# First two units of the linear attention: level blocks of 64 keys, one unit two levels ahead of the other, decays on VectorE, x from PSUM

## The reference

```
for t in range(S):
    state = alpha[:, :, t, :, None] * state + np.einsum('bhd,bhe->bhde', k[:, :, t], v[:, :, t])
    y[:, :, t] = np.einsum('bhd,bhde->bhe', q[:, :, t], state)
...
h = x @ w_in                                   # 384 -> 2048
g = np.where(h > 0.0, h, alpha * (np.exp(np.minimum(h, 0.0)) - 1.0))
x = g @ w_out                                  # 2048 -> 384
...
p = domain_probs / (domain_probs.sum(-1, keepdims=True) + 1e-09)
for e in range(E):                             # 4 experts, 384 -> 1024 -> 384
    out += p[:, e:e + 1] * (np.maximum(x @ w1[e], 0.0) @ w2[e])
```

## Time and profile before

| | |
|---|---|
| Time, median of 3 | 1351.81 us |
| Profiled execution, its time | 1348.95 us |
| Its span | 1347.2 us |
| TensorE busy | 1296.9 us (96%) |
| VectorE / ScalarE / GpSimd busy | 832.6 / 605.9 / 564.3 us |
| TensorE in the 40 slices of the span | 2589999999999999999999999999999999999998 |

### The profile page before, as it was taken

The page is one execution under the profiler, slowest core; times in us unless marked ns, Lnnn a source line. Parts: engine busy times, 40 slices in busy tenths (PEclk is TensorE's granted clock), DMA queues, the critical chain, the costliest instruction groups (busy, mean ns, idle before and its releaser), DMA issues.

```text
span 1347.2 us, 27542 instructions
## 1 busy us (share of the span) xinstructions
PE 1296.9 (96%) x11112; PEld 1067.4 (79%) x11112; DVE 832.6 (62%) x1097; ACT 605.9 (45%) x1043; POOL 564.3 (42%) x485
## 2 busy tenths in 40 slices
PE   2589999999999999999999999999999999999998
PEld 2568788888888888888888888888888888888886
DVE  2478676675576766567676567666647654654443
ACT  0456534347534336733435753434754433653331
POOL 5574384840353861174691164484035321100012
PEclk9999999999999999999999999999999999999999
DMA  6054435236435335524424533523643333433330
GB/s 229 20 165 156 132 107 163 75 102 188 140 106 196 87 98 164 170 85 141 151 83 125 178 117 110 168 90 100 189 141 106 99 87 94 148 94 102 98 95 23
DMA packets 87682, 165.84 MB, mean 123 GB/s; under 512 B 30338, under 2 KB 35843, under 8 KB 87556
## 3 DMA queue, kind: packets, MB, share of 16 engines
q1 hardware_dynamic: 87556, 164.08, 39.4%
HBM read 157.97 MB, written 6.08 MB: 122 GB/s over the span
## 4 chain that ended last, share of the span: by engine, by line
PE 90%; issue 6%; DVE 1%; POOL 1%; DMA 0%; ACT 0%; SPq 0%; POOLq 0%; DVEq 0%; ACTq 0%
PE ps_o L563 14%; PE ps_h L563 14%; PE ps_o L564 14%; PE ps_o L565 14%; PE ps_h L564 14%; PE ps_h L565 14%; PE ps_att L438 2%; PE ps_att L532 1%; POOL acc L1075 1%; PE ps_att L508 1%; PE ps_att L536 1%; PE ps_att L490 1%; PE ps_att L541 1%; DMA alpha<-in_a 0%; PE ps_o L470 0%
## 5 line engine op out<-in xcount | busy, mean ns | idle before, releaser
L726 DVE TENSOR_TENSOR w_lo<-w_stage,w_hi 128x768 fp32r<-128x768 f32 x288 | 340.2, 1181 | 30.8 <-ACT w_hi L894 27.1
L563 PE MATMUL ps_o<-g_hi,w_lo 128*128 128x512 f32 x864 | 342.5, 396 | 0.7 <-DVE g_lo L742 0.7
L563 PE MATMUL ps_h<-x_hi,w_lo 128*128 128x512 f32 x864 | 338.2, 391 | 4.4 <-DVE x_lo L732 3.8
L921 ACT ACTIVATE g_hi<-ps_h 128x512 fp32r<-128x512 f32 x192 | 114.8, 598 | 500.0 <-PE ps_h L565 499.9
L564 PE MATMUL ps_h<-x_lo,w_hi 128*128 128x512 f32 x864 | 337.0, 390 | 0.0
L565 PE MATMUL ps_h<-x_hi,w_hi 128*128 128x512 f32 x864 | 337.0, 390 | 0.0
L564 PE MATMUL ps_o<-g_lo,w_hi 128*128 128x512 f32 x864 | 336.7, 390 | 0.0
L565 PE MATMUL ps_o<-g_hi,w_hi 128*128 128x512 f32 x864 | 336.6, 390 | 0.0
L746 DVE SCALAR_TENSOR_TENSOR g_lo<-ps_h,g_hi 128x512 fp32r<-128x512 f32 x192 | 132.3, 689 | 262.8 <-ACT g_hi L921 262.6
L894 ACT CAST w_hi<-w_stage 128x768 fp32r<-128x768 f32 x288 | 239.4, 832 | 1.0
L272 POOL TENSOR_TENSOR products<-blocks 128x384 f32<-128x384 f32 x150 | 194.8, 1312 | 90.6 <-DVE scores L673 88.2
(11 more groups left out here) (104 smaller groups left out, 1002.9 us busy)
## 6 DMA issues: line engine op xcount, KB each, us to landing
w_stage<-in_w SPq DMA_DIRECT2D x288, 384.0 KB, 3.1
alpha<-in_a SPq DMA_DIRECT2D x12, 512.0 KB, 4.2
v_tok<-in_v SPq DMA_DIRECT2D x12, 512.0 KB, 5.7
p_rows<-p_norm SPq DMA_DIRECT2D x6, 1024.0 KB, 9.3
k_level<-in_k SPq DMA_DIRECT2D x10, 512.0 KB, 5.7
q_low<-in_q SPq DMA_DIRECT2D x10, 512.0 KB, 6.5
out<-acc SPq DMA_DIRECT2D x18, 256.0 KB, 3.9
blocks<-in_q_blocks SPq DMA_DIRECT2D x10, 384.0 KB, 3.8
```

Source lines behind the costliest of these rows:

```text
L563: nc.tensor.matmul(dst, lhs[1], rhs[0], start=first, stop=False)
L726: nc.vector.tensor_tensor(wl[n % WRING][:], stage[n % STAGE][:], wh[n % WRING][:].bitcast(F32), ALU.subtract).then_inc(w_low, 1)
L921: nc.scalar.activation(gh[n % GS][:], ps_h[n % 2][:], ACT.Relu).then_inc(g_hi, 1)
```

## The change

It rewrites what stands ahead of the first step, for units 0 and 1:

- Levels 0 to 5 multiply blocks of 64 keys with 32 queries each: 32 matmuls for a level of a unit, where levels 0 to 4 had 64 of 32 keys with 16 queries. Level 6 stays. Levels 0 to 3 are masked into `near` on VectorE; levels 4 and 5 are copied into `near` by ScalarE (`early_rect`), and `near`, now in blocks of 64, goes to the pair weights in two copies a unit. `near` moves from the `products` buffer to the `blocks` buffer.
- The order is `EARLY_ORDER`: unit 0 is two levels ahead of unit 1. Semaphores are split by unit. `transpose_k(0)`, `outer(0)`, `attend(0)` stand among the last levels of unit 1; `first_state` comes first.
- The decays of units 0 and 1 move from GpSimd (`totals`) to VectorE (`early_totals`).
- `to_x` falls away for tile 0: `high_x` and `lower_x` read the attention's PSUM bank.
- Loads: q and k of a unit in one DMA each; the first key and value, masks and identity on ScalarE's queue; the blocks of unit 2 wait for `near` to be free and come after `load_unit(2)`.

```diff
-MASKED = 5
+MASKED = 4
...
-def early(u, l):
-
-    return LEAD * l + u + 1
-
+
+EARLY_ORDER = [(0, 0), (0, 1)]
+for lag in range(LEVELS - 2):
+    EARLY_ORDER += [(0, lag + 2), (1, lag)]
+EARLY_ORDER += [(1, LEVELS - 2), (1, LEVELS - 1)]
...
             def load_blocks(u):
                 if u > LEAD:
                     sp.wait_ge(prod, NPROD * (u - LEAD))
+                else:
+                    sp.wait_ge(e_near, LEAD)
...
+            load_unit(LEAD)
             load_blocks(LEAD)
-            load_unit(LEAD)
...
             def load_early(u):
-                for c in range(2):
-                    t = slice(P * c, P * (c + 1))
-                    sp.dma_start(KL[u][:, :, t], k_d[u][:, :, t]).then_inc(e_in[u], 16)
-                    sp.dma_start(QT[u][:, :, t], q_d[u][:, :, t]).then_inc(e_in[u], 16)
+                sp.dma_start(KL[u][:], k_d[u]).then_inc(e_in[u], 16)
+                sp.dma_start(QT[u][:], q_d[u]).then_inc(e_in[u], 16)
...
-                        for m in range(P // COL):
-                            t = slice(P * c + COL * m, P * c + COL * (m + 1))
+                        for j in range(2):
+                            t = slice(P * c + HALF * j, P * c + HALF * (j + 1))
                             for sd in range(2):
                                 r = slice(HALF * sd, HALF * (sd + 1))
                                 right = QT[u][r, pr, t].rearrange("p (n two h) -> p n two h", two=2, h=1 << l)[:, :, 1, :]
-                                last = nc.tensor.matmul(banks[sd][COL * m:COL * (m + 1), SUB * (PAIRS * c + pr):SUB * (PAIRS * c + pr + 1)],
+                                last = nc.tensor.matmul(banks[sd][HALF * j:HALF * (j + 1), COL * (PAIRS * c + pr):COL * (PAIRS * c + pr + 1)],
                                                         KL[u][r, pr, t], right, start=True, stop=True)
...
-            for l in range(LEVELS):
-                for u in range(LEAD):
-                    early_pairs(u, l)
+            first_state()
+            for u, l in EARLY_ORDER[:-2]:
+                early_pairs(u, l)
             pe.wait_ge(eye_in, 16)
             transpose_k(0)
             transpose_k(1)
-            first_state()
+            early_pairs(1, LEVELS - 2)
+            outer(0)
+            early_pairs(1, LEVELS - 1)
+            attend(0)
             transpose_k(2)
             transpose_k(3)
-            outer(0)
-            attend(0)
+            attend(1)
             outer(1)
-            for g in range(1, EARLY):
-                attend(g)
+            attend(2)
+            attend(3)
...
+            def early_totals(u, l):
+                if l == 0:
+                    dve.wait_ge(a_in[u], 16)
+                else:
+                    dve.wait_ge(e_td[u], l)
+                halves = TD[l][u][:].rearrange("p a (m two) -> p a m two", two=2)
+                nc.vector.tensor_tensor(TD[l + 1][u][:], halves[:, :, :, 0], halves[:, :, :, 1], ALU.mult).then_inc(e_td[u], 1)
...
+            for u, l in EARLY_ORDER:
+                early_queries(u, l)
+                early_totals(u, l)
+                if l < MASKED:
+                    early_masked(u, l)
+                if (u, l) == (1, LEVELS - 3):
+                    lower_w(0)
...
+            def early_rect(u, l):
+
+                h = 1 << l
+                act.wait_ge(e_step[u], l + 1)
+                if l == LEVELS - 1:
+                    act.wait_ge(cleared, CLEARS)
+                    for sd in range(2):
+                        for dst, src in rectangles(ps_l[l % 2][u], weights[u], l, sd):
+                            last = nc.scalar.copy(dst, src)
+                else:
+                    if l == MASKED:
+                        act.wait_ge(e_mask[u], MASKED)
+                    for sd in range(2):
+                        dst = near[:, u].rearrange("p (a s) t -> p s a t", s=2)[:, sd]
+                        src = ps_l[l % 2][u][sd][:, 0:HEADS * COL].rearrange("p (a t) -> p a t", a=HEADS)
+                        for m in range(HALF // h):
+                            rows, n = slice(2 * m * h, (2 * m + 1) * h), m % (COL // h)
+                            last = nc.scalar.copy(dst[rows, :, (2 * n + 1) * h:(2 * n + 2) * h], src[rows, :, n * h:(n + 1) * h])
+                last.then_inc(e_rect[u], 1)
...
-            for l in range(LEVELS):
-                totals(0, l)
-            for l in range(LEVELS):
-                early_keys(0, l)
-                totals(1, l)
-                early_keys(1, l)
-            for g in range(EARLY):
+            for u, l in EARLY_ORDER:
+                early_keys(u, l)
+                if (u, l) == (1, LEVELS - 2):
+                    decay_state(0)
+            for g in range(1, EARLY):
                 decay_state(g)
```

More of the change, by code:

```diff
@@ L184, in program @@
         part = sbs("part", 2, [P, TILE])
-        mk = sb("masks", [P, MASKED, SUB])
+        mk = sb("masks", [P, MASKED, COL])
         k0 = part[0][0:1, :].rearrange("p (a t) -> p a t", a=PAIRS)
@@ L189, in program @@
         weights = [PW[:], early_w]
-        near = prods[:].rearrange("p r x -> p (r x)")[:, 0:2 * 2 * HEADS * COL].rearrange("p (u a t) -> p u a t", u=2, a=2 * HEADS)
+        near = blocks[:].rearrange("p r x -> p (r x)")[:, 0:2 * 2 * HEADS * HALF].rearrange("p (u a t) -> p u a t", u=2, a=2 * HEADS)
         ps_a = ps("ps_att", BANKS)
@@ L452, in early_pairs @@
                 if l == 0:
-                    pe.wait_ge(e_in[u], 64)
+                    pe.wait_ge(e_in[u], 32)
                 else:
-                    pe.wait_ge(e_q, early(u, l - 1))
-                    pe.wait_ge(e_k, early(u, l - 1))
-                if l >= 2:
-                    pe.wait_ge(e_mask, early(u, l - 2))
+                    pe.wait_ge(e_q[u], l)
+                    pe.wait_ge(e_k[u], l)
+                if 2 <= l < MASKED + 2:
+                    pe.wait_ge(e_mask[u], l - 1)
+                elif l >= MASKED + 2:
+                    pe.wait_ge(e_rect[u], l - 1 - MASKED)
+                if u == 1 and l == 1:
+                    pe.wait_ge(st_ready, 1)
                 banks = ps_l[l % 2][u]
-                if l >= MASKED:
-                    level(banks, u, l).then_inc(e_step, 1)
+                if l == LEVELS - 1:
+                    level(banks, u, l).then_inc(e_step[u], 1)
                     return
@@ L495, in outer @@
                 if u < LEAD:
-                    pe.wait_ge(e_rect, early(u, LEVELS - 1 - MASKED))
+                    pe.wait_ge(e_rect[u], LEVELS - MASKED)
                 else:
@@ L931, in high_x2 @@
                     nc.scalar.copy(x2[0][:, m, :], ps_o[m][:]).then_inc(x2_hi, 1)
-            for u in range(LEAD):
-                early_near(u)
-            for l in range(MASKED, LEVELS):
-                for u in range(LEAD):
-                    early_place(u, l)
+            act.dma_start(k0, k0_d).then_inc(first_in, 16)
+            act.dma_start(v0, v0_d).then_inc(first_in, 16)
+            act.dma_start(mk[:], masks_d).then_inc(masks_in, 16)
+            act.dma_start(eye[:], eye_d).then_inc(eye_in, 16)
+            early_rect(0, MASKED)
+            high_w(0)
+            early_rect(0, MASKED + 1)
+            high_w(1)
+            early_rect(1, MASKED)
+            early_near(0)
+            early_rect(0, LEVELS - 1)
             k_tokens(0)
             k_tokens(1)
-            high_w(0)
+            early_rect(1, MASKED + 1)
+            early_near(1)
+            high_w(2)
+            early_rect(1, LEVELS - 1)
             k_tokens(2)
             k_tokens(3)
-            high_w(1)
-            to_x(0)
             high_x(0)
-            high_w(2)
-            to_x(1)
-            high_x(1)
             high_w(3)
-            to_x(2)
-            high_x(2)
-            to_x(3)
-            high_x(3)
+            for g in range(1, EARLY):
+                high_x(g)
             for n in range(AHEAD):
@@ L1142 @@
     step = np.arange(P)
-    masks = np.zeros((P, MASKED, SUB), np.float32)
-    near = np.arange(COL)
+    masks = np.zeros((P, MASKED, COL), np.float32)
+    near = np.arange(HALF)
     for l in range(MASKED):
@@ L1147 @@
         right = near[(near // h) % 2 == 1]
-        masks[:, l] = step[:, None] % COL // h == right[None, :] // h - 1
+        masks[:, l] = step[:, None] % HALF // h == right[None, :] // h - 1
     ins = {"q": q_l, "k": k_l, "a": a_l, "v": v_l,
```

135 lines of the change are left out of this document (66 added, 69 removed).

## The result

The changed kernel takes 1329.34 us (median of four runs, 1328.66 to 1331.01), and the kernel before, beside it, 1352.63 us (1351.22 to 1353.86). The ratio is 0.983, with a 95% interval of 0.9813 to 0.9847, 23.3 us less. Forecast were 1330 us and the range 1322 to 1340.

What follows compares the result with a forecast made beforehand. TensorE was taken as the bound, 96% busy, with only the start to win: first step at 53.1 us instead of 74.9, so 1348.95 - 21.8 = 1327.15, plus 2.86 to the median, 1330 us; range 1322 to 1340.

Steps and rivals of the forecast that it cites:

- The bound and the mechanism: Ahead of the first step TensorE waits for packets of 256 instructions, 3.76 us each; halving matmuls of levels removes five packets.
- The levels: Early levels of units 0 and 1: products of level 4 of unit 1 end at 32.3 us (29 to 37).
- The burst: TensorE's 64 matmuls of the new form for one level of one unit: 0.9 to 2.1 us, taken as 1.2.
- packets set the pace: Per step of the new level order, TensorE's packet takes 3.76 us, a little longer than GpSimd's 3.3 and VectorE's work.
- The decay on VectorE: Decays in the early levels, two per step on VectorE, the largest about 0.3 us.
- The loads: Start of the kernel: fewer DMAs give first products at 6.2 us and their key update's end at 7.6.
- ScalarE's queue: From level 4 of unit 1, ScalarE sets the pace: 6.8 us to 39.1, then 7.3 to 46.4.
- The clock: Half clock stays in the first steps; ahead of them half of the last two `attend`'s doubling adds 1.1 us.
- the slow end: Levels end at 37 us, all `attend` fully doubled (+2.3 us), first step at 60 to 61 us: 1338 us.
- A delay per level: Rival: a hidden 2.3 us follows every early level, so the body starts at 73 to 74 us: 1349 to 1351; 4%.
- The rival that VectorE and GpSimd become the bound: In the early levels a step takes 5 us, not 3.76; start near 64 us, 1341 us; 7%.
- Blocks of unit 2: Loads landing 1 to 2 us into the body cost nothing; rival: over 15 us in, TensorE waits, kernel slower, 3%.

Runs made afterwards that it cites:

- double: The kernel before, with each matmul of levels 0 to 4 of units 0 and 1 issued twice in a row: 1391.24 us (before beside it 1352.79).
- blocks32: The changed kernel with levels 2 to 4 of units 0 and 1 in blocks of 32 keys and 16 queries again: 1337.26 us.
- rect5: The changed kernel with level 5 multiplied for only the 32 left keys of each block of 64: 1329.55 us.
- x_tile: The changed kernel with x of tile 0 copied to an SBUF buffer first, as before: 1331.89 us.
- late_decays: The changed kernel with each level's decay behind its masked copies on VectorE, not ahead of them: 1328.29 us.
- old_loads: The changed kernel with q and k loaded in halves and masks, identity, first key and value on SP's queue, as before: 1331.28 us.
- act_order: The changed kernel with ScalarE doing unit 0's near and last rectangles ahead of unit 1's level 4, second weight cast one place earlier: 1326.39 us.
- level_order: The changed kernel with the old order of levels on all engines (unit 0, unit 1, next level): 1330.01 us.

## Why the prediction was right

**The bound and the mechanism.** That the gaps are packets of 256 instructions, and that halving the matmuls of a level takes them away, was right: double and blocks32 show it from both sides. The instruction queue of the changed kernel moves 1.36 MB in 83 packets over the span, five fewer than the 88 of before, as forecast; 9 stand ahead of the first step, where 14 stood.

**The levels: off by 3.6 us.** Products of (1,4) were to end at 32.3 us and ended at 35.9. Up to (1,1) the forecast held: its burst was to begin at 20.7 us and began at 20.57. From there the forecast had three packets, 11.3 us, and 0.3 us of the last burst. Two things were wrong.

- The burst is the term that was mis-sized, 1.2 us forecast ("nearer the one with equal columns") and 1.93 measured. I chose the wrong row: the 64x64 row with 33 ns a matmul was the near one, since the time goes with the width of the weights (rect5). The last burst alone costs 1.6 us more than its 0.3.
- That packets set the pace did not hold. The five bursts and level 6 between the start of (1,1) and (1,4) are 10.8 us of work, less than the packets' 11.3, but they took 13.3: TensorE waited 2.7 us for VectorE and GpSimd, in five gaps of 0.15 to 1.00 us, which the forecast had at nothing. In x_tile the same stretch took 11.9 us, so most of these waits differ from one execution to the next.

The decay on VectorE, forecast at up to 0.3 us, took 1.0 to 2.0 beside a key update. The key update was no longer for it (1.99 us with the decay beside it, 2.00 in late_decays); it is the decay that waits, with what stands behind it on VectorE. No run gives this a price that is clear of the executions' own differences. The key updates took 1.05 to 1.99 us, 1.5 in the mean (forecast 1.65). The forecast took its lower row, the 1.50 us at 13.42 us of before, for one beside VectorE; VectorE was idle there until 15.36.

**The loads** gave the first update at 8.5 us, forecast 7.6; old_loads puts their worth at some 2 us, in the start and in the median (1331.28 and 1329.34).

**ScalarE's queue: right up to `k_tok` of unit 0.** From (1,4) to the first step 20.8 us were forecast and 19.9 measured. The single terms hold: 8 copies 2.1 us (forecast 1.9), two near copies 2.1 (2.3), rectangles 1.5, `k_tok` 1.07. The 0.5 us of semaphores in the sum rest on no row; the pauses between the end of `attend(3)` and the first step come to 0.20 us. ScalarE runs without a pause from 35.89 until it ends `k_tok` of unit 1 at 49.75, as forecast. But the chain leaves it at 42.43 and goes through TensorE, partly at half clock, which ends `attend(1)` at 49.87: the two tie. act_order shows that the queue was the limit up to 42.43, since a new order of the same copies gives 2.45 us.

**The clock: wrong in its place, small in size.** I had the half clock of the first steps stay. It went, 1.2 us, because x from PSUM makes the idle time before them 1.72 us and not 3.8; with x from `x_tile` it is 3.33, and the half clock is back. Inside the stage the forecast had 1.1 us, for the two last `attend`. No run shows these two doubled, nor all four, as the 2.3 us of the slow end have it: they took 1.74 us each at a granted clock of 1.00, `attend(1)` as much, and `attend(0)`, at 0.65, took 2.59. The half clock came from 43.0 to 46.4 us, on level 6 of unit 1 and `attend(0)`, and this work took 1.3 us longer than in act_order. So the size was right and the place was not.

**The sum.** The first step was 2.7 us late (55.79, forecast 53.1), the first steps 1.2 us quicker and the body 0.6 us longer. The profiled execution was forecast at 1327.15 and took 1329.32. The median comes out at 1330 by the 2.86 us added for the distance of before's profiled execution from its median, which the changed kernel doesn't have (1329.32 and 1329.34): two errors of opposite sign, each near 2 to 3 us. That the median is met within 1 us is luck; that the range is met is not.

**The rivals.** A delay per level is refuted (double). Its own sum in the forecast was off: 12 levels of 3.76 us from 9.2, and 20.7 behind them, make 75 us, not 73 to 74. The rival that VectorE and GpSimd become the bound had 5 us a step for the forecast's 3.76. Measured from (1,1) to (1,4) are 4.4 us a step in the changed kernel's profile and 4.0 in x_tile's: these two engines do end TensorE's waits, but 5 us a step were not reached. Blocks of unit 2 began 2.3 us into the body. TensorE's second wait in the body, 0.6 us, comes at 121 us, 65 us in; its cause was not looked into. A cost of these blocks was not seen. That the lead of two levels matters was assumed in the forecast and not priced apart; level_order shows no worth of it that can be told from nothing.

## What to carry to other kernels

When TensorE stops with nothing to wait for, first see that no update ended just ahead ("issue" stood for a wait of GpSimd twice here), then count the instructions between two stops: if it is the same number each time (254 to 256 here), fewer and larger matmuls are worth more than a better order (7.3 us of start in blocks32, 2.1 in level_order). Price a small matmul by the width of its weights and not by its moving columns alone (1.93 us for 64 of them with 64-wide weights, 1.08 with 32-wide ones, 32 columns in both). An engine that copies results in program order, here ScalarE, should not have finished work of one unit queued behind a wait for the other (2.45 us in act_order). A few us of idle time ahead of dense work cost again behind it here, by the clock: 1.4 us in x_tile's first steps behind 3.33 us, 1.3 us on (1,6) and `attend(0)` of the changed kernel behind 2.78. And before a place in one profile is put down to an edit, look at a stretch that the edit leaves alone: here such a stretch moved by 1.5 us.

## What the runs showed of the hardware

- Packets of instructions: 3.4 to 4.2 us from one burst of TensorE to the next (before, double, blocks32), whatever the work in them (1.43 us of matmuls before, 1.78 in double), 4.2 to 6.2 us under loads.
- 64 matmuls with 64-wide weights and 32 moving columns took 1.93 us, with 32-wide weights 1.08.
- The ten decays on VectorE that start inside a key update of GpSimd in the changed kernel end 0.03 to 0.55 us after it: the first takes 1.98 us, against 0.75 in late_decays, and the one of level 3 takes 1.33 us when it starts 0.04 us behind the key update, against 0.20 in act_order, 0.23 us ahead of it.
- The last two subtractions of x took 1.02 us with x in PSUM and 2.30 with x in SBUF, GpSimd working beside both.
- Half clock in the first steps went with 3.33 us (x_tile), 3.62 us (double) and 3.81 us (before) of idle time ahead of them (granted clock 0.82, 0.70 and 0.79 over the first 27 matmuls), full clock with 1.72 us or less. Ahead of the outer products 2.78 us went with a clock of 0.50 from 43.0 to 46.4 us and 2.59 us for `attend(0)` (changed kernel); 2.79 us in x_tile with 2.89 us for it, though the granted clock reads 1.00 there; in act_order `attend(0)` took 1.74.
